# Fused attention and two MoE layers on one core: x loaded by heads, VectorE's products in front of the lower parts, another GpSimd order in step 0

## What is computed

```python
attn = softmax(mask(q @ k.T / 8)) @ v            # 4 x 8 x 576 x 64
x = attn.transpose(0, 2, 1, 3).reshape(2304, 512)
h = x @ w_in;  x = (h * clip(h + 3, 0, 6) / 6) @ w_out          # 512 -> 2048 -> 512
h = x @ w_in2; y = (h * tanh(softplus(h))) @ w_out2
```

## Time and profile before

| | |
|---|---|
| median of 3 runs | 977.72 us (974.49 to 978.66) |
| profiled execution, its own time | 975.95 us |
| its span, first to last instruction | 974.0 us |
| granted TensorE clock, mean | 0.998 of full speed |
| TensorE (PE) busy | 952.0 us, 98% |
| VectorE (DVE) | 746.6 us, 77% |
| ScalarE (ACT) | 643.6 us, 66% |
| GpSimd (POOL) | 431.3 us, 44% |
| DMA | 216.42 MB, mean 222 GB/s |

### The profile page before, as it was taken

The page is one execution under the profiler, slowest core; times in us unless marked ns, Lnnn a source line. Parts: engine busy times, 40 slices in busy tenths (PEclk is TensorE's granted clock), DMA queues, the critical chain, the costliest instruction groups (busy, mean ns, idle before and its releaser), DMA issues.

```text
span 974.0 us, 17754 instructions
## 1 busy us (share of the span) xinstructions
PE 952.0 (98%) x6028; PEld 848.0 (87%) x6028; DVE 746.6 (77%) x1417; ACT 643.6 (66%) x1431; POOL 431.3 (44%) x410
## 2 busy tenths in 40 slices
PE   8999999999999999999899999999999999999998
PEld 7898888999887888888788988998998988988896
DVE  7898898774868686789788787777887777777654
ACT  7999999754544445454445557777777777776663
POOL 7899779665837596776867670000000000000000
PEclk9999999999999999999999999999999999999999
DMA  7988898657698978788786546555655654565255
GB/s 217 270 240 243 258 273 234 173 153 238 220 291 291 290 256 252 234 294 252 269 275 212 209 170 217 176 202 195 215 197 184 231 210 155 182 248 187 90 193 194
DMA packets 84601, 216.42 MB, mean 222 GB/s; under 512 B 10144, under 2 KB 16928, under 8 KB 84512
## 3 DMA queue, kind: packets, MB, share of 16 engines
q1 hardware_dynamic: 84368, 215.01, 67.6%
q10 hardware_dynamic: 144, 0.29, 0.1%
HBM read 162.07 MB, written 39.92 MB: 207 GB/s over the span
## 4 chain that ended last, share of the span: by engine, by line
PE 67%; DVE 7%; DMA 6%; SPq 4%; POOL 3%; issue 2%; ACT 1%; ACTq 0%; DVEq 0%; POOLq 0%
PE psum L1021 32%; PE psum L904 10%; PE psum L906 10%; PE psum L905 10%; DMA ext_d<-ext_made 3%; PE psum L849 2%; PE psum L828 2%; DVE ebuf L1624 1%; PE psum L808 1%; POOL osplit L1885 1%; SPq L646 1%; DVE glo L1630 1%; PE psum L809 1%; SPq L648 1%; DVE ext_made L1530 1%
## 5 line engine op out<-in xcount | busy, mean ns | idle before, releaser
L1021 PE MATMUL psum<-ghi,osplit 128*128 128x512 f32 (+1 forms) x640 | 216.7, 372 | 2.1 <-POOL osplit L1885 2.1
L904 PE MATMUL psum<-xhi,whi 128*128 128x256 f32 (+1 forms) x640 | 188.0, 294 | 5.1 <-ACT snap L1242 2.5
L906 PE MATMUL psum<-xhi,wlo 128*128 128x256 f32 (+1 forms) x640 | 187.2, 293 | 0.0
L905 PE MATMUL psum<-xlo,whi 128*128 128x256 f32 (+1 forms) x640 | 187.0, 292 | 0.0
L1021 PE MATMUL psum<-osplit,ghi 128*128 128x512 f32 x576 | 180.7, 395 | 1.3 <-DVE glo L1630 1.3
L1630 DVE SCALAR_TENSOR_TENSOR glo<-ebuf,ghi 128x512 fp32r<-128x512 f32 x144 | 126.5, 878 | 22.9 <-ACT ghi L1290 14.8
L904 PEld LDWEIGHTS psum<-xhi,whi 128*128 128x128 f32 x640 | 121.1, 189 | 19.0 <-ACT snap L1242 4.4
L1290 ACT ACTIVATE ghi<-ebuf 128x512 fp32r<-128x512 f32 x144 | 90.4, 628 | 66.9 <-DVE ebuf L1624 46.2
L1021 PEld LDWEIGHTS psum<-ghi,osplit 128*128 128x128 f32 x640 | 118.5, 190 | 18.4 <-issue 2.7
L1885 POOL TENSOR_TENSOR osplit<-oraw,osplit 128x512 fp32r<-128x512 f32 x80 | 117.2, 1468 | 38.1 <-ACT osplit L1209 34.0
L905 PEld LDWEIGHTS psum<-xlo,whi 128*128 128x128 f32 x640 | 121.2, 189 | 10.5
(11 more groups left out here) (120 smaller groups left out, 2147.4 us busy)
## 6 DMA issues: line engine op xcount, KB each, us to landing
ext<-ext_d SPq DMA_DIRECT2D x56, 768.0 KB, 4.4
osplit<-o_d SPq DMA_DIRECT2D x80, 512.0 KB, 5.3
oraw<-in_w_out SPq DMA_DIRECT2D x80, 256.0 KB, 5.8
wraw<-in_w_in SPq DMA_DIRECT2D x26, 512.0 KB, 6.0
ext_d<-ext_made SPq DMA_DIRECT2D x32, 384.0 KB, 6.2
attn_t<-ostage SPq DMA_DIRECT2D x32, 288.0 KB, 3.7
qkin<-in_qk SPq DMA_DIRECT2D x30, 288.0 KB, 3.7
kparts<-kparts SPq DMA_DIRECT2D x30, 288.0 KB, 4.2
```

Of the source, the lines that this page charges most:

```text
L904: pe.matmul(dst, hi, xh, start=(start and cc == 0), stop=False, skip_group_check=True)
L905: pe.matmul(dst, hi, xl, start=False, stop=False, skip_group_check=True)
L906: last = pe.matmul(dst, lo, xh, start=False, stop=(stop and cc == 1), skip_group_check=True)
L1021: last = pe.matmul(bank(Y_BANK + c, n), stat, mov, start=(first and m == 0), stop=(final and m == 2), skip_group_check=True)
```

## The change

Four things are changed. The order of all TensorE and ScalarE work stays.

1. **x by heads, with fewer DMAs.** For blocks 1 to 4 a half of x takes six DMAs in place of eight: per side (one of two heads of each chunk) two DMAs of attention output and one of both chunks' reciprocals. The bytes are the same. For block 1's first half the two sides go out in attention steps 27 and 29 (before: four parts in 27 to 30).
2. **Where they stand on SyncE.** For blocks 2 to 4 side 0 is issued near the start of its step, before the load of extra operands, `wraw` and the raw W_out tiles; side 1 stays where the whole load was.
3. **VectorE's order** in layer one: products with h and the first lower part of g come before the lower parts of the extra operands and of W_out.
4. **GpSimd's order in step 0**: the next W_out tile is split before block 1's second half is mixed.

```diff
 X_LOADS = [[sum(16 * n(b) for b in range(blk)) for blk in range(NBLK + 1)] for n in (
-    lambda b: (16 if KIND[b] == SHORT else 8) if b < NBL else 1,
-    lambda b: 0 if KIND[b] == SHORT else 8 if b < NBL else 2 if b > NBL else 1)]
+    lambda b: (16 if KIND[b] == SHORT else 6) if b < NBL else 1,
+    lambda b: 0 if KIND[b] == SHORT else 6 if b < NBL else 2 if b > NBL else 1)]
...
-EARLY_X_LOAD, NEXT_X_LOAD = tuple(range(11, 19)), (27, 28, 29, 30)
+EARLY_X_LOAD, NEXT_X_LOAD = tuple(range(11, 19)), (27, 29)
...
+            def load_x_side(x, cc, h, cols, done):
+                rows = slice(h * DH, (h + 1) * DH)
+                for i in range(2):
+                    sp.dma_start(x[rows, i, 0:2, :],
+                                 attn_t[4 * i + 2 * cc + h, :, cols].rearrange("(s d) t -> d s t", s=2)
+                                 ).then_inc(done, 16)
+                rinvs = r_d[2 * cc + h:HEADS:4, cols]
+                sp.dma_start(x[rows, :, 2, :], rinvs.unsqueeze(0).broadcast_to([DH, 2, cols.stop - cols.start])
+                             ).then_inc(done, 16)
...
-            def next_x(s):
+            def next_x(s, side):
                 for blk in range(2, LATE_X):
                     t = s - (FIRST_STEP[blk] - 2)
-                    if t == -8:
-                        load_x(blk, 0)
-                    if t == -4 and KIND[blk] == QUAD:
-                        load_x(blk, 1)
+                    sides = (side,) if blk < NBL else range(2 * side)
+                    if t == -8 and sides:
+                        load_x(blk, 0, sides)
+                    if t == -4 and sides and KIND[blk] == QUAD:
+                        load_x(blk, 1, sides)
+                if side == 0:
+                    return
...
                 for t in ahead_at(s - 1):
                     store_ahead_hi(t)
+                next_x(s, 0)
                 if quad(s + 3):
                     load_ext(s + 3)
...
-                next_x(s)
+                next_x(s, 1)
...
-                extra_jobs(s - 1)
-                ahead_os(s - 1)
                 relu6_times_h(s + 1, 0)
                 relu6_times_h(s + 1, 1)
                 split_g_lo(s + 1, 0)
+                extra_jobs(s - 1)
+                ahead_os(s - 1)
                 mixing_jobs(s)
...
                 if s == 0:
                     add_x(1, 3)
                     scale_x(1, 3)
-                    mix_x(1, 1)
                 next_x(s, 0)
                 for i in todo[1:2]:
                     split_o(i)
+                if s == 0:
+                    mix_x(1, 1)
                 next_x(s, 1)
```

More of the change, by code:

```diff
@@ L650, in load_x_chunk, with load_x @@
                                  ).then_inc(done, 16)
-            def load_x(blk, cc):
+            def load_x_side(x, cc, h, cols, done):
[7 more added lines that the diff above has]
+                             ).then_inc(done, 16)
+            def load_x(blk, cc, sides=range(2)):
                 t0 = first_token(blk)
@@ L660, in load_x @@
                     attention_stored(-(-cols.stop // SEQ))
-                    for i in range(2):
-                        load_x_chunk(x_staged(blk, cc, i), 2 * i + cc, cols, x_loaded[cc])
+                    for h in sides:
+                        load_x_side(xst_late if blk == 1 and cc == 1 else xst, cc, h, cols, x_loaded[cc])
                     return
@@ L731, in _ @@
                 if n in NEXT_X_LOAD:
-                    i, side = divmod(NEXT_X_LOAD.index(n), 2)
-                    if i == 0 and side == 0:
+                    if n == NEXT_X_LOAD[0]:
                         sp.wait_ge(x_lo, X_SPLITS[1])
                         attention_stored(2)
-                    load_x_chunk(x_staged(1, 0, i), 2 * i, slice(HT, HT + TB), x_loaded[0], (side,))
+                    load_x_side(xst, 0, NEXT_X_LOAD.index(n), slice(HT, HT + TB), x_loaded[0])
                 if in_use(n) and n != LAST:
```

## The result

| | before | changed |
|---|---|---|
| median of 20 runs each, one chip | 976.27 us (973.08 to 979.27) | 979.6 us (976.52 to 984.14) |
| ratio, 95% interval | | 1.0038 (1.0025 to 1.0051) |
| profiled execution, span | 974.0 us | 978.8 us |
| its mean granted clock | 0.998 | 0.994 |
| end of attention (PE's first instruction behind its last wait there) | 184.76 us | 186.31 us |

The account below looks back on a forecast made before the run. PE, busy 952.0 of 974.0 us, bounds the kernel; 12 us of waits and slow clock were winnable. Terms -3.4 - 1.5 - 0.3 - 4.0 - 1.0 + 1.0 = -9.2 from 975.95 gave 966.8, plus 0.7: 967.5 us, range 964 to 974.5.

Parts of the forecast that it names:

- the sentence on queues: Loads of wraw and raw tiles: held back some 3 us by VectorE's later side work, hidden if wraw lands before next mixing.
- GpSimd's order in step 0: PE near 211 us: the 2.1 us wait and 1.7 us of slow clock go, 0.4 us wait left; -3.4 us.
- VectorE's order, steps 19 to 27: PE's waits from 392 to 503 us: of 5.4 us due to VectorE, all but 1.4 go; -4.0 us.
- the 2.3 of step 24: PE's third product in step 24: its 2.3 us wait for ScalarE's copy goes whole with VectorE's products in front.
- I keep 1.4 of the 5.4: Steps 19 to 27: 1.4 us of VectorE's 5.4 us of waits stay, since without idle time moving changes nothing.
- VectorE's order, steps 4 to 11: Products PE awaits at 317.6 us come 1.5 us sooner, -1.5; the similar wait between 318 and 392 us, -0.3.
- x by heads: GpSimd's wait for x: block 3's 1.0 us PE wait goes, -1.0; block 4 gets a new one, +1.0.
- Half of x now starts behind the store, 3.5 us before the old start: Step 22: half of x goes out ahead of the load at 446.59, 3.5 us before the old start at 450.08.
- GpSimd's wait for x in step 23: Sign of being right: this wait, 7.61 us before, becomes shorter by 3 us.
- it starts where the mixing started: GpSimd in step 0: the moved W_out split starts at 208.82 and is ready at 210.5, so no wait.
- x and GpSimd take over: Rival, chance 0.2: x lands no earlier and GpSimd's chain holds PE; only 4.4 us gained, 972.3 as a median.
- Slower: Rival, chance 0.07: lower part always in front of add_c12 makes 16 steps 0.99 us longer each; 983 us.

Follow-up runs that it names:

- e1: Kernel before with VectorE's new order alone (products in front of the two lower parts): 981.9 us, ratio 1.0062 (1.0042 to 1.0081).
- e2: Kernel before with GpSimd's new order in step 0 alone: 975.6 us, ratio 0.9992 (0.9974 to 1.0009).
- e7: Kernel before with VectorE's new order only in steps 20, 21 and 23 to 27: 974.2 us, ratio 0.9998 (0.9977 to 1.0018).
- e3: Kernel before with x in six DMAs and side 0 early, VectorE's and GpSimd's order as before: 977.8 us, ratio 1.0019 (1.0003 to 1.0035).
- e12: Changed kernel with VectorE's new order in steps 20 to 27 only, the old one before: 978.1 us, ratio to kernel before 1.0022 (1.0002 to 1.0042).
- e4: Changed kernel with both sides of x issued where the whole load stood: 984.8 us, ratio to kernel before 1.0091 (1.0073 to 1.0109).
- e9: Kernel before with VectorE's new order in step 14 alone: 978.5 us, ratio 1.0027 (1.0005 to 1.0048).
- e5: Kernel before with VectorE's new order, and SyncE's wraw and W_out loads and lower-part stores behind x and raw tiles: 985.9 us, ratio 1.0086 (1.0056 to 1.0116).
- e15: Same kernel as e11, measured once more against the kernel before: 972.4 us, ratio 0.9968 (0.9945 to 0.9992).
- e11: Kernel before with e7's VectorE order and GpSimd's lower parts of x before W_out splits in steps 9, 17, 25: 972.2 us, ratio 0.9976 (0.9952 to 1.0000).
- e6: Kernel before with only the extra operands' lower part behind VectorE's products, W_out's staying in front: 988.2 us, ratio 1.0109 (1.0085 to 1.0133).

## Why the prediction was wrong

The step that failed is the sentence on queues that put the later lower parts at nothing. On it rest the terms for VectorE's order, -5.8 us in all; e1 measured +6. The term for GpSimd's order in step 0, -3.4, failed too; e2 measured no gain clear of noise. Part by part:

**VectorE's order, steps 19 to 27 (-4.0):** right in itself. The waits from 430 to 492 us fell from 5.4 to 1.0, the 2.3 of step 24 went whole, and no product of VectorE waited for a store any more. "I keep 1.4 of the 5.4" was even too careful. But most of it was not kept: with VectorE's part alone in these steps block 4's x is late by 1.59 us, the clock takes 1.5 us more a run, and the ratio is 0.9998 (e7).

**VectorE's order, steps 4 to 11 (-1.5, -0.3):** the wait went from 1.46 to 0.76; not 1.5. The step that failed stands in the text on queues: "Later products of VectorE's side work also hold `wraw` and raw tiles back by some 3 us; this is hidden as long as `wraw` lands before the next mixing". I looked at who needs `wraw`, and not at who stands behind its load. In the changed kernel that is, in step 3, VectorE's lower part at 242.33 and SyncE's load behind it, in front of a raw tile that ScalarE needs before it can copy y (the kernel before issued this load at 235.54):

```profile
244.14 0.33 SPq L620 DMA_DIRECT2D hbuf<-in_w_out  x1
244.51 0.43 SPq L611 DMA_DIRECT2D oraw<-in_w_out  x1
```

and in steps 6 and 14 it is x. The raw tile's delay is not needed for the gap of 1.71 us near 250, though: with x by heads and VectorE's old order there it is 1.95 (e3) and 1.97 (e12), with VectorE's new order alone 0.79 (e1). The "some 3 us" was about right: e1's 5 to 6 us in step 14 are 3.5 to 4 once PE's own lateness is taken off. What was wrong is "hidden".

**x by heads (-1.0 and +1.0):** Block 3's wait was to go and is 3.08, though with VectorE's old order it is gone (e3) or 0.78 (e12); block 4's was to be 1.0 and is 1.59 (e7 has the same 1.59 with x as before, so this one is the term I had, PE being early for it). "Half of x now starts behind the store, 3.5 us before the old start" took from the list when the load may go, and did not ask what it waits for. SyncE and GpSimd in step 14 of the changed kernel:

```profile
359.00 0.33 SPq L624 DMA_DIRECT2D o_d<-staged  x1
363.22 1.24 SPq L655 DMA_DIRECT2D xst<-attn_t  x2
...
365.79 0.43 SPq L620 DMA_DIRECT2D wraw<-in_w_out  x1
...
367.82 1.24 SPq L655 DMA_DIRECT2D xst<-attn_t  x2
```

```profile
360.02 3.18 POOL L1885 TENSOR_TENSOR xlo<-xst,xhi 128x512 fp32r<-128x512 f32 x2
...
378.54 1.29 POOL L1848 TENSOR_TENSOR xst<-xst 128x512 f32<-128x512 f32 x1 [3.46 <-DMA xst<-r_d]
```

There is one `xst`, and the second half of x cannot be loaded before GpSimd has split the first half's lower parts, at 363.20. SyncE stood at this load for 4 us with everything behind it. In step 22 side 0 started at 452.39 (the old start was 450.08). By the rows of the kernel before the buffer was no obstacle:

```profile
355.80 2.99 POOL L1872 TENSOR_TENSOR xlo<-xst,xhi 128x512 fp32r<-128x512 f32 x2
...
443.38 3.17 POOL L1872 TENSOR_TENSOR xlo<-xst,xhi 128x512 fp32r<-128x512 f32 x2
```

There GpSimd was done with the first half at 358.79 and 446.55, just when side 0 was to go out. In the changed kernel it is done at 363.20 and 452.37, 4.4 and 5.8 us later, and in e1, with x loaded as before, at 363.22 in step 14. So this lateness of GpSimd is there with VectorE's order alone, without the early side. The 4 us of standing also cost less than 4: the load of `wraw` behind it had to wait for VectorE's lower part, which ended at 364.76, and went out at 365.79. The Trainium skill (DMA: Bandwidth & Descriptors, "Anatomy of one DMA — SWDGE (gpsimd) path") says that any semaphore wait happens on the issuing sequencer, before the DMA is handed on; the section is about DMAs that GpSimd issues, the sentence is general. By that rule all that stands behind is held up too, and the trace agrees, with 4 us at this load. Still the early side was right for this order of VectorE's: without it x is later yet (e4).

**GpSimd's wait for x in step 23** shrank from 7.61 us to 2.88, which I had named as a sign of being right. It was none: GpSimd started on x at 468.34, 3.75 us later than before. Its wait was short because GpSimd itself came to it late.

**GpSimd's order in step 0 (-3.4):** the clock stayed full, the wait was 1.05 and another 0.36. The step "it starts where the mixing started" left out that the moved split needs ScalarE's upper part:

```profile
211.53 1.79 POOL L1898 TENSOR_TENSOR osplit<-oraw,osplit 128x512 fp32r<-128x512 f32 x1 [2.04 <-ACT osplit L1222]
```

Alone this part measures 0.9992 (e2). In full, the kernel before loses 1.2 to 1.8 us a run to the clock wherever its waits fall, and of its executions in these comparisons a third to two fifths show 1.000. The wait of 2.10 us and the slow stretch behind it were not the usual case. Of twelve profiles with GpSimd's old order here only one more, e9, has them (2.10 us, then 0.50 from 218 to 220); the other ten wait 0.92 to 1.49 us and keep a full clock. The five with the new order wait 1.33 to 1.56 us in two parts. So against an ordinary execution there was nothing to win.

**The rivals.** "Slower" had the lower part in front of `add_c12` as its mechanism; in the changed kernel that did not happen (1.0 us behind `snap_3`, 2.5 before), it did in e5 (8.1), and with the same order of VectorE's to a lesser degree in e1 (3.4) and e4 (4.0). "x and GpSimd take over" named the right engine and called it a smaller gain. What I had no case for is that VectorE's order makes x late, and that the wait then takes the clock with it.

**Attention** ended 1.5 us later in the changed kernel's profile. This is not the change's: PE's products of the row sums stand at 145.50 us in place of 143.93, 1.6 us late already, and the first load of x in the new form goes out at 169.13. Between 99 and 145 us PE waited 1.5 us behind what the profile calls issue, before 0.3. Why it waited there stays open. Profiles with x by heads end attention at 184.8 to 186.7 us, others at 184.6 to 188.4; the two at 188.3 and 188.4 (e9, e15) have a clock of 0.79 to 0.87 between 125 and 135 us.

## What to carry over

When work without a hurry is moved behind work with one, follow its outputs into the other engines' queues: who waits for them there, and what stands behind that wait. A load's place in a list says when it can go at the earliest; the buffer that it fills says when it does. And a kernel whose engines take turns at being late may give nothing for one removed wait, since the next in line takes its place. A wait of 2 to 3 us can cost twice its length: the windows around the one of 3.08 us, at 0.92, 0.50 and 0.89, lose (0.08 + 0.50 + 0.11) x 5 = 3.5 us to the clock. Read the same wait in more than one profile before counting it as gained.

## What the hardware showed that I had not expected

- **The clock falls behind some short waits and not behind other, longer ones.** It was at half behind 3.08 us at 405 us (changed kernel), fell to 0.66 behind 1.59 at 496 us, and to 0.67 behind 1.87 at 376 us (e3); it stayed full behind 2.3 at 474 us (kernel before) and behind 2.79 at 316 us (e1). So in these profiles the length of the wait alone does not tell whether the clock falls. What it costs, the mean clock of every run measures: from 0.8 us a run (e11) to 8.2 (e6).
- **Profiles of one kernel differ by more than the effects looked for.** e11's and e15's are the same kernel: spans of 969.1 and 974.9 us, attention's end at 185.12 and 188.44, and in e15's a clock of 0.85 and 0.81 from 125 to 135 us. One profile gives the mechanism; for 2 us only the repeated runs give the sign.
